# A hand-written order around two layers: mixing u blocks into the v tiles, and w_out loaded to its own place

## The reference

```python
def _moe_ref(x, w_tok1, w_tok2, w_ch1, w_ch2):
    xt = x.transpose(0, 2, 1)
    h = np.maximum(xt @ w_tok1, 0.0) @ w_tok2
    u = x + h.transpose(0, 2, 1)
    h2 = np.maximum(u @ w_ch1, 0.0) @ w_ch2
    return u + h2

def _moe2_ref(x, w_in, w_spatial, b_spatial, w_out):
    h = np.maximum(x @ w_in, 0.0)
    u, v = (h[..., :d_ff // 2], h[..., d_ff // 2:])          # d_ff = 1024
    v_n = (v - mean(v)) / np.sqrt(var(v) + 1e-06)            # over the last axis
    v_s = np.einsum('ts,bsd->btd', w_spatial, v_n) + b_spatial[None, :, None]
    return (u * v_s) @ w_out
```

## Time and profile before

| | |
|---|---|
| median of 3 runs | 471.54 us (471.33 to 471.81) |
| the profiled execution's own time | 471.33 us |
| its span, first to last instruction | 469.5 us |
| PE busy | 463.1 us (99% of the span) |
| PEld busy | 393.5 us (84%) |
| DVE busy | 187.6 us (40%) |
| ACT busy | 157.0 us (33%) |
| POOL busy | 130.8 us (28%) |
| mean granted TensorE clock | 0.999 of full speed |

### The profile page before, as it was taken

How to read it: one execution, slowest core, us unless ns; L and a number is a source line. 1 busy time by engine, 2 the same in 40 slices (tenths; PEclk the granted TensorE clock), 3 DMA queues, 4 the chain that set the end, 5 groups by cost and what they waited for, 6 DMA issues and landing times.

```text
span 469.5 us, 6968 instructions
## 1 busy us (share of the span) xinstructions
PE 463.1 (99%) x2620; PEld 393.5 (84%) x2620; DVE 187.6 (40%) x521; ACT 157.0 (33%) x415; POOL 130.8 (28%) x145
## 2 busy tenths in 40 slices
PE   7999999999999999999999999999999999999997
PEld 3777777899888888888888888888999898899985
DVE  7889898236411211511113211106872045214220
ACT  4988887247211110311111212204612123312112
POOL 5377863324132221400002222223850003300000
PEclk9999999999999999999999999999999999999999
DMA  8577674036121111000000011101000100100012
GB/s 317 180 280 289 227 269 148 26 94 194 58 82 45 46 45 46 0 1 0 0 1 0 2 45 45 46 22 34 1 1 0 68 0 1 67 1 1 1 45 89
DMA packets 13906, 33.10 MB, mean 70 GB/s; under 512 B 1584, under 2 KB 3248, under 8 KB 13872
## 3 DMA queue, kind: packets, MB, share of 16 engines
q1 hardware_dynamic: 13584, 31.86, 20.0%
q10 hardware_dynamic: 288, 0.79, 0.4%
HBM read 29.49 MB, written 3.15 MB: 70 GB/s over the span
## 4 chain that ended last, share of the span: by engine, by line
PE 97%; DVE 1%; ACT 1%; DMA 1%; issue 0%; ACTq 0%; DVEq 0%
PE ps L386 27%; PE ps L387 27%; PE ps L388 27%; PE ps L1079 6%; PE ps L1121 5%; PE ps L1093 4%; PE ps L1192 1%; DMA n_words<-in_n_both 1%; ACT prob L605 0%; DVE prob L845 0%; DVE bias L821 0%; DVE probT L853 0%; ACT out_sb L747 0%; ACT oT L618 0%; DVE dist L816 0%
## 5 line engine op out<-in xcount | busy, mean ns | idle before, releaser
L1013 DVE SCALAR_TENSOR_TENSOR R_l<-ps,R_h 128x512 fp32r<-128x512 f32 x36 | 24.9, 692 | 134.9 <-ACT R_h L682 134.9
L682 ACT ACTIVATE R_h<-ps 128x512 fp32r<-128x512 f32 x36 | 21.4, 595 | 130.5 <-PE ps L388 130.5
L388 PE MATMUL ps<-UT_h,wc_l 128*128 128x512 f32 x144 | 56.0, 389 | 0.0
L387 PE MATMUL ps<-UT_l,wc_h 128*128 128x512 f32 x144 | 56.0, 389 | 0.0
L386 PE MATMUL ps<-UT_h,wc_h 128*128 128x512 f32 x144 | 56.0, 389 | 0.0
L605 ACT ACTIVATE prob<-prob,neg_max 128x256 f32<-128x256 f32 (+1 forms) x96 | 45.8, 480 | 4.5 <-DVE neg_max L845 4.4
L386 PE MATMUL ps<-R_h,wc2a 128*128 128x512 f32 x96 | 37.3, 389 | 0.0
L387 PE MATMUL ps<-R_l,wc2a 128*128 128x512 f32 x96 | 37.3, 389 | 0.0
L388 PE MATMUL ps<-R_h,wc2a 128*128 128x512 f32 x96 | 37.3, 389 | 0.0
L569 POOL TENSOR_TENSOR UT_l<-xsum,UT_h 128x512 fp32r<-128x512 f32 x12 | 16.8, 1410 | 71.8 <-ACT UT_h L673 71.8
L845 DVE CUSTOM_DVE_ANT_0 prob<-ps,bias 128x256 f32<-128x256 f32 (+1 forms) x96 | 33.6, 390 | 0.8 <-PE ps L1093 0.5
(11 more groups left out here) (134 smaller groups left out, 1001.6 us busy)
## 6 DMA issues: line engine op xcount, KB each, us to landing
vv<-in_v_pairs SPq DMA_DIRECT2D x8, 768.0 KB, 4.5
kk<-in_k_pairs SPq DMA_DIRECT2D x7, 768.0 KB, 7.8
staged<-in_moe_w_ch SPq DMA_DIRECT2D x20, 256.0 KB, 2.9
out<-out_sb SPq DMA_DIRECT2D x12, 256.0 KB, 2.0
qT<-in_q_pairs SPq DMA_DIRECT2D x7, 384.0 KB, 6.5
staged<-in_moe_w_spatial SPq DMA_DIRECT2D x9, 256.0 KB, 2.7
staged<-in_moe_w_in SPq DMA_DIRECT2D x8, 256.0 KB, 2.6
staged<-in_moe_w_tok SPq DMA_DIRECT2D x6, 256.0 KB, 5.2
```

Of the source, the lines that this page charges most:

```text
L387: pe.matmul(o, a[0], b[1], start=False, stop=False, skip_group_check=True)
L388: return pe.matmul(o, a[1], b[0], start=False, stop=stop, skip_group_check=True)
L682: act.activation(R[0][:, f % 3, :], ps[:, 4 + f % 4, :], ACT.Relu).then_inc(ring_hi, 1)
L1013: dve.scalar_tensor_tensor(out=R[1][:, f % 3, :], in0=ps[:, 4 + f % 4, :], scalar=0.0, in1=R[0][:, f % 3, :].bitcast(F32), op0=ALU.max, op ...
```

## The change

TensorE now takes u0 after v2 and u1 after v4. ACT, DVE and POOL all follow one string, `ORDER`, in which x1, x2 and x3 stand later than before and the last piece of w_spatial stands first. "s" in it is a step of the normalization: on ACT the square root of tile i and the high part of tile i-1, on POOL the low part of tile i-1, and on DVE, for i = 6, the last norm. Pieces of w_out no longer go through the ring of slots. SP loads them to places of their own (`wo_raw`, over the memory of `gT1` and of w_ch1) once the last hidden product of the channel layer is done. DVE and POOL split them behind the steps s3, s4, s5 and s6 instead of after the whole string. ACT's first write to `gT1` waits for these splits.

```diff
@@ buffers @@
+            wo_raw.append(region(at_x + (18 + 24 * i) * KB)(f"wo_raw{i}", [P, 3, D], F32))
@@ early, landed, slot @@
-            return TOK_END <= s < EARLY_END
+            return TOK_END <= s < EARLY_END or s >= WSP_END
+            if s >= WSP_END:
+                return wo_landed[s - WSP_END]
+            if s >= WSP_END:
+                return wo_raw[(s - WSP_END) // 3][:, (s - WSP_END) % 3, :]
@@ orders @@
-        ORDER_PE = order("v0 v1 v2 v3 v4 v5 u0 u1 u2 u3")
-        ORDER_ACT = order("v0 w8 q0 v1 x0 q1 h0 v2 x1 q2 h1 v3 x2 q3 h2 v4 x3 q4 h3 v5 u0 q5 h4 u1 h5 u2 u3")
-        ORDER_DVE = order("v0 x0 v1 x1 v2 x2 v3 x3 v4 v5 v6")
-        ORDER_POOL = order("x0 h0 x1 h1 x2 h2 x3 h3 h4 h5")
+        ORDER_PE = order("v0 v1 v2 u0 v3 v4 u1 v5 u2 u3")
+        ORDER = order("w8 v0 s0 v1 x0 s1 v2 s2 x1 v3 u0 s3 v4 s4 v5 u1 s5 s6 u2 x2 u3 x3")
+        ORDER_V1 = order("v0 s0 v1 s1 v2 s2 v3 s3 v4 s4 v5 s5 s6")
@@ SP @@
-            for s in range(WSP, WO_END):
+            for s in range(WSP, WSP_END):
+                load_piece(sp, s)
+            sp.wait_ge(ring_ready, 2 * B * DB + FB * NCH)
+            for s in range(WSP_END, WO_END):
                 load_piece(sp, s)
@@ POOL @@
-            for kind, i in ORDER_POOL:
-                if kind == "h":
-                    vn_lo_part(0, i)
-                if kind == "x":
-                    x2_lo_part(NCH - 1, i, X2_LAST[i])
-            for s in range(WSP_END, WO_END):
-                split_lo(pool, s)
-            for t in range(NT):
-                vn_lo_part(1, t)
+            for b in range(B):
+                for kind, i in (ORDER if b == 0 else ORDER_V1):
+                    if kind == "s" and i > 0:
+                        vn_lo_part(b, i - 1)
+                    if kind == "x":
+                        x2_lo_part(NCH - 1, i, X2_LAST[i])
+                    if b == 0 and kind == "s" and i in (3, 4, 5, 6):
+                        split_lo(pool, WSP_END + i - 3)
@@ ACT (v_root is folded into v_std, which keeps its order for the second batch) @@
+                    if n == 0:
+                        wait_lo(act, WO_END - 1)
+                        wait_hi(act, WO_END - 1)
-            for kind, i in ORDER_ACT:
+            for kind, i in ORDER:
@@ DVE @@
-            for kind, i in ORDER_DVE:
-                if kind == "v":
+            for kind, i in ORDER:
+                if kind == "v" or (kind, i) == ("s", NT):
                     v_tile(0, i)
                 if kind == "x":
                     x2_part(NCH - 1, i, X2_LAST[i])
-            for s in range(WSP_END, WO_END):
-                split_hi(dve, s)
+                if kind == "s" and i in (3, 4, 5, 6):
+                    split_hi(dve, WSP_END + i - 3)
```

More of the change, by code:

```diff
@@ L100, in build @@
         out_sb = xr("out_sb", [P, 2, D], F32)
-        wsp, gT1 = [], []
+        wsp, gT1, wo_raw = [], [], []
         for i, x in enumerate("hl"):
@@ L227, in build @@
         x2_lo = sem("x2_lo")
+        wo_landed = [sem(f"wo_landed{i}") for i in range(GB)]
         b_landed = sem("b_landed")
@@ L696, in v_tile @@
                     act.activation(V32[:, n % 3, :], ps[:, 4 + n % 2, :], ACT.Relu).then_inc(vv_relu, 1)
-            def v_root(b, t):
-                act.wait_ge(vv_var, b * NT + t + 1)
-                act.activation(std[:, t % 2, 1:2], std[:, t % 2, 0:1], ACT.Sqrt).then_inc(vv_std, 1)
             def v_std(b, t):
+                n = b * NT + t
                 if t < NT:
-                    v_root(b, t)
+                    act.wait_ge(vv_var, n + 1)
+                    act.activation(std[:, t % 2, 1:2], std[:, t % 2, 0:1], ACT.Sqrt).then_inc(vv_std, 1)
                 if t > 0:
@@ L751, in y_part @@
                     y_tile((2 * b + half) * (NT // 2) + t)
-            for kind, i in ORDER_ACT:
+            for kind, i in ORDER:
                 if kind == "v":
                     v_tile(0, i)
[L756 to L759, removed]
+                if kind == "s":
+                    v_std(0, i)
                 if kind == "x":
```

## The result

| | before | changed |
|---|---|---|
| median of 6 runs | 471.56 us (471.33 to 472.23) | 476.07 us (475.12 to 477.65) |
| profiled execution, span | 471.33, 469.5 us | 476.14, 474.1 us |
| granted TensorE clock, mean | 0.999 | 0.995 |

The ratio is 1.0089 (95% interval 1.0072 to 1.0106). A second measurement of the same changed kernel gave 475.50 us and 1.0060 (1.0039 to 1.0081). The sign and both of the named waits came as forecast. The median is 2.2 us above the forecast of 473.9 and 0.2 us above the upper end of the range.

What follows compares the result with a forecast made beforehand. TensorE was taken to bound the kernel, busy without a wait from 83 to 466 us. Losses of 0.37 and 2.2 us, 2.6 in sum, on the execution's 471.33 gave 473.9 us, with an 8-in-10 range of 472.2 to 475.9.

Steps and rivals of the forecast that it cites:

- both of the named waits: TensorE waiting for x0's first step near 325.7 (0.3 to 1 us) and x2's near 342.5 (1 to 4 us).
- TensorE has nothing to gain there: In the stretch of the change TensorE has no wait to remove, and every added wait goes straight to the end.
- u0: 0.37 us: TensorE's loss before u0, as x0's first step stands behind DVE's turn for v1; bounds 0.13 and 1.12 us.
- The first spatial product: 2.2 us: TensorE's loss before that product, as x2's first step stands late on DVE; bounds 0.3 and 4.0 us.
- the four lengths: On DVE ahead of x2: v4's norm 1.30, third cast 0.42, last norm 0.55, fourth cast 1.51 us.
- Later needs at 0: After the first spatial product starts, x3, v5's low part and gT's first write come in time; 1 us of cover.
- rival A: DVE's line from v4's norm to x2: port mostly free, not slower, 472.0 to 472.5 us; 15%.
- TensorE's order at 0: On TensorE after u0, the reordered blocks u1, v3 to v5, u2 and u3 find their inputs in time; cost 0.
- The w_out loads, last piece of w_spatial first: 0: Loads land some 14 us before use, and the w_spatial piece fills time when ACT waits for v0; cost 0.
- the granted clock 1.00 throughout: Expected sign in the trace after: TensorE's granted clock never falls.
- rival C: Clock falls in the stall, the first spatial product's 18 matmuls run at half rate: another 3.1 us, 477.0 us; 6%.
- The sum of 2.6 us: Total predicted loss: 0.37 us at u0 plus 2.2 us before the first spatial product.

Runs made afterwards that it cites:

- b1: Kernel before with one added wait: TensorE takes the first spatial product only once POOL has w_out's second low part; 474.73 us, ratio 1.0053.
- c1: Changed kernel with w_out's splits moved behind the gating steps and x0 ahead of v1 in the one string; 472.18 us, ratio 0.9995.
- a2: Changed kernel with w_out's casts moved behind DVE's gating steps and its low parts behind POOL's string, x2 and x3 left late; 472.38 us, ratio 1.0002.
- a1: Changed kernel with x2 moved ahead of v5 on DVE alone; 476.23 us, ratio 1.0077.
- a3: Kernel before with TensorE's new order alone, the relus of u0 and u1 moved along on ACT; 472.57 us, ratio 1.0008.
- a0: Changed kernel measured again with no edit; 475.50 us, ratio 1.0060.
- b2: Kernel before with one added wait: TensorE takes the first spatial product only once POOL has w_out's third low part; 477.83 us, ratio 1.0115.
- b3: Kernel before with one added wait: TensorE takes the first spatial product only once POOL has w_out's fourth low part; 479.32 us, ratio 1.0138.
- c2: Changed kernel with x0 to x3 in the first four turns, w_out's splits still behind s3 to s6; 479.88 us, ratio 1.0145.

## Why the prediction was right in kind and short in size

- **TensorE has nothing to gain there.** Right. No run had fewer waits in the stretch than the kernel before, and an added wait of 2.06 us went to the end whole (b1).
- **u0: 0.37 us.** Measured 0.34 (0.26 of delay, 0.08 in the matmul behind it). The restart took 0.15 us where 0.24 had been put. The chain came out as worked: norm 0.52 with POOL idle (0.55 taken). c1 shows the cause: x0's place.
- **The first spatial product: 2.2 us.** Measured 2.35. Of the four lengths on which it rests, v4's norm was put at 1.30 and took 1.51. The third cast (0.42), last norm (0.55) and fourth cast (1.51) took 0.41, 0.55 and 1.49. a2 shows that the held norm and the fourth cast make the wait. The two that came behind a POOL instruction were held, the two that started with POOL idle were not, as the Trainium skill's rule cited with the earlier trace rows has it. One reading there was off: "a POOL instruction and a short cast" would be 1.28 + 0.42 = 1.70 us, and the cast took 1.51. In the traces a held instruction ends 0.28 to 0.29 us behind POOL's, less than its whole free length.
- **Later needs at 0.** Right. v5's low part ended at 347.12 and was wanted at 345.17 + 15 x 0.174 = 347.78: 0.7 us of cover where 1 had been put. That POOL's line is the next wait if the first one goes stands in rival A, at 0.3 to 0.8 us. In a1 it cost 2.4 us (126.16 - 123.78), with two of its subtractions stretched to 1.74 and 1.71 us beside DVE.
- **TensorE's order at 0.** 0.13 us too low (a3, c1).
- **The w_out loads, last piece of w_spatial first: 0.** Right. The four loads went out together at 309.75 and landed in 3.6 us each (2.6 in the earlier trace rows), 20 us ahead of the first cast.
- **The failed step is "the granted clock 1.00 throughout"**: rival C, held at 6% because the wait was shorter than the 2.6 us of the earlier trace rows. In the profiled execution it happened and cost 1.58 us (3.1 had been put). It isn't certain per execution: of 32 executions of the changed kernel 18 had a low mean clock, of 56 of the kernel before 22, and that difference may be chance. So it isn't shown that this wait makes falls more frequent. Over all 32 executions of the changed kernel the median is 475.9, over all 56 of before 472.1. Where the clock was up throughout they are 474.96 and 471.78, 3.2 us apart, of which 2.84 are traced. The other 0.3 to 0.4 lies outside the traced part. v0's start moves between 317.45 and 318.3 at full clock in kernels with the same attention, so it may lie there. Against the kernel before of the same measurement, clock up on both sides, such a rest is 0.2 us for a0 (3.03 against 2.84) and 0.5 for b1 (2.72 against 2.18), which has nothing but one added wait, so it need not come from the change. Its cause is left open.

The sum of 2.6 us was thus within 0.3 of what is traced at full clock (2.84). The other 1.9 of the 2.2 us by which the forecast fell short have three parts. It was added to the profiled execution's 471.33, near the fastest of its kernel, where executions with the clock up have a median of 471.78: 0.45. The unexplained rest is 0.3. And the low clock in half of the six executions makes up the last 1.1 (476.07 against 474.96).

## What to carry to other kernels

Where the bounding engine has no wait, a new order can only cost: look up what each engine's string puts ahead of the instruction that frees its next buffer, and give that the earliest place. When a wait is taken away, work out the deadline of every other input of the same product first, as the second latest may be almost as late. And price a wait of TensorE of some 2 us or more with a possible low clock behind it. Here that was 1.6 us, behind a wait of 2.35 us in one of two traces and behind 3.4 and 4.7 us in both.

## What was not expected of the hardware

- The clock fell 0.3 to 1.5 us after a wait had ended (changed kernel, b2, b3, c2), and stayed at half for 3.4 us while matmuls ran. The cost is paid in work: 0.32 instead of 0.174 us between matmuls of 384 columns.
- The same fall came at 10.4 to 11.1 us, in the attention, in three of the profiled executions (a0, a2, b3), whose attention is that of the kernel before. That the 22 of 56 executions of the kernel before with a low mean clock (473.2 instead of 471.8 us) fell there too fits, but no trace of one was seen.
- After a wait the second matmul also started late, by 0.07 to 0.11 us.
